# The turns of w_out and the gates' folds inside the first block's steps, and an opening with long products: linear attention and two expert layers on one core

## The reference

```python
for t in range(S):                       # B=4, H=8, S=768, D=48
    cur = np.einsum('bhd,bhe->bhde', u[None] * kt, vt)
    y[:, :, t] = np.einsum('bhd,bhde->bhe', rt, state + cur)
    state = w[None, :, :, None] * state + np.einsum('bhd,bhe->bhde', kt, vt)
x = y as 3072 tokens x 384
h = max(x @ w1, x @ w2, x @ w3)          # 384 -> 768
x = h @ w_out                            # 768 -> 384
logits = x @ w_gate;  noisy = logits + log1p(exp(x @ w_noise)) * noise
top 2 of 8 experts, softmax over the two; out += weight * relu(x @ ew1[e]) @ ew2[e]
```

## Time and profile before

| | us |
|---|---|
| median of 3 runs | 889.2 |
| the profiled execution, its own time | 889.12 |
| its span | 887.2 |
| TensorE busy | 872.6 (98%) |
| VectorE busy | 451.0 (51%) |
| ScalarE busy | 271.2 (31%) |
| POOL busy | 385.2 (43%) |
| mean granted clock of TensorE | 0.994 |

### The profile page before, as it was taken

How to read it: one execution, slowest core, us unless ns; L and a number is a source line. 1 busy time by engine, 2 the same in 40 slices (tenths; PEclk the granted TensorE clock), 3 DMA queues, 4 the chain that set the end, 5 groups by cost and what they waited for, 6 DMA issues and landing times. The chain is left out here.

```text
span 887.2 us, 19589 instructions
## 1 busy us (share of the span) xinstructions
PE 872.6 (98%) x6566; PEld 855.1 (96%) x6567; DVE 451.0 (51%) x1100; ACT 271.2 (31%) x520; POOL 385.2 (43%) x380
## 2 busy tenths in 40 slices
PE   7999999999999999999999999999999999999996
PEld 6999999999999999999999999999999999999996
DVE  6675555636564564646573564352525335264322
ACT  3442322223231233215314342331414233143210
POOL 5245244244253534325444555454534435355442
PEclk9899999999999999999999999999999999999999
DMA  9595212222122221023215622624326252442221
GB/s 229 132 293 138 68 51 64 60 58 58 57 57 61 57 64 37 2 92 97 46 46 190 176 77 50 187 61 142 116 60 199 70 180 73 137 135 69 64 78 52
DMA packets 103765, 86.08 MB, mean 97 GB/s; under 512 B 60634, under 2 KB 93090, under 8 KB 103696
## 3 DMA queue, kind: packets, MB, share of 16 engines
q1 hardware_dynamic: 82704, 31.56, 15.0%
q0 software_dynamic: 12416, 26.28, 9.6%
q10 hardware_dynamic: 8576, 27.33, 9.5%
HBM read 70.46 MB, written 21.35 MB: 103 GB/s over the span
## 5 line engine op out<-in xcount | busy, mean ns | idle before, releaser
L1413 PE MATMUL ps<-yh,wh 128*128 128x384 f32 x432 | 148.7, 344 | 1.7 <-ACT x_sb L1196 1.3
L1304 ACT ACTIVATE gh<-ps 128x384 fp32r<-128x384 f32 x136 | 66.9, 492 | 264.6 <-PE ps L1415 264.6
L1415 PE MATMUL ps<-yh,wl 128*128 128x384 f32 x432 | 145.5, 337 | 0.0
L1414 PE MATMUL ps<-yl,wh 128*128 128x384 f32 x432 | 145.4, 337 | 0.0
L1413 PE MATMUL ps<-xgh,w1h 128*128 128x384 f32 (+1 forms) x456 | 145.0, 318 | 0.0
L1415 PE MATMUL ps<-xgh,w1l 128*128 128x384 f32 (+1 forms) x456 | 145.0, 318 | 0.0
L1414 PE MATMUL ps<-xgl,w1h 128*128 128x384 f32 (+1 forms) x456 | 144.9, 318 | 0.0
L1060 DVE SCALAR_TENSOR_TENSOR gl<-ps,gh 128x384 fp32r<-128x384 f32 x136 | 75.8, 557 | 126.8 <-ACT gh L1304 126.8
L1413 PE MATMUL ps<-w2h,gh 128*128 128x384 f32 x408 | 138.2, 339 | 0.6 <-DVE gl L1054 0.6
L1414 PE MATMUL ps<-w2l,gh 128*128 128x384 f32 x408 | 136.5, 335 | 0.0
L1415 PE MATMUL ps<-w2h,gl 128*128 128x384 f32 x408 | 136.5, 335 | 0.0
(11 more groups left out here) (200 smaller groups left out, 1497.1 us busy)
## 6 DMA issues: line engine op xcount, KB each, us to landing
ew_raw<-ew ACTq DMA_DIRECT2D x28, 768.0 KB, 4.6
v_sb<-vN SPq DMA_DIRECT2D x24, 192.0 KB, 3.3
out<-zrow SPq DMA_DIRECT2D x1, 4608.0 KB, 16.3
x_rows<-x_sb ACTq DMA_DIRECT2D x8, 576.0 KB, 3.6
kn_sb<-kN SPq DMA_DIRECT2D x20, 192.0 KB, 2.8
k_raw<-kT SPq DMA_DIRECT2D x48, 72.0 KB, 2.7
wraw<-moe_w SPq DMA_DIRECT2D x6, 576.0 KB, 6.9
e_raw<-ew SPq DMA_DIRECT2D x4, 768.0 KB, 5.0
```

The source lines that it names most:

```text
L1304: act.activation(gh[:, f, :], ps[f % 4][:, 0:T], ACT.Relu).then_inc(gh_ok, 1)
L1413: pe.matmul(o, ah, bh, start=start, stop=False)
L1414: pe.matmul(o, ah, bl, start=False, stop=False)
L1415: return pe.matmul(o, al, bh, start=False, stop=stop)
```

## The change

1. The opening's 22 transposes of the identity become 4 products of 384 columns: the identity by `state[0]`, which POOL has cleared, so the result is zero. Three transposes follow, and further groups of 4, 3, 8, 6 and 6 are put between the chunks' parts. `keep_turning` now takes a bank.
2. `turn_wo(0)` moves from behind the second own sums to the end of the opening, `turn_wo(1)` behind the first block's step 0. Both use banks 7, 6 and 3. ScalarE keeps the second half in step 0, behind the first maxima, and TensorE waits for all six parts (`wo_ok`) behind step 1.
3. Both folds move behind the block's step 3 (bank 6, beyond column 384), ScalarE's copy and split of them with them, VectorE's `fold_low` from behind step 3 to behind step 4.
4. SyncE's queue loads the first three weight pieces ahead of w_out. The first piece is split earlier: by ScalarE ahead of its parts of y, by VectorE between the second and third chunk's rows.
5. The third chunk's own sums stand ahead of the second outputs, on TensorE and VectorE.
6. Buffers are laid out in another order in SBUF; no size changes.

```diff
 TURN = (6, 7, 0)
-FOLD = 1
+WO_TURN = (7, 6, 3)
+FOLD = 6
...
+            for q in range(BS):
+                load_piece(q)
             for n in range(2):
                 at = 3 * KD * F1 + n * PW
                 sp.dma_start(wo_raw[n][:, :, :].rearrange("p f n -> p (f n)"), moe_w[:, at:at + PW]).then_inc(wo_in[n], 16)
-            for q in range(BS):
-                load_piece(q)
...
                 if first:
-                    fold_low(0)
-                    fold_low(1)
                     split_wo_low(0)
...
                 if first:
+                    fold_low(0)
+                    fold_low(1)
                     split_wo_low(1)
...
             masks(0, 2)
+            own_weights(0, 2)
             states(0, 1)
             rows_of_y(0, 1)
-            own_weights(0, 2)
             split_y_low(0, 0, 3)
+            split_piece_low(0)
             rows_of_y(0, 2)
             split_y_low(0, 1, 4)
             split_y_low(0, 2, 0)
-            split_piece_low(0)
             states(0, 2)
...
-                    if first and f == 2:
+                    if first and f == 0:
+                        keep_turned(1)
+                    if first and f == 3:
+                        keep_folded()
                         split_fold_high(0)
                         split_fold_high(1)
...
             fade(0, 1)
-            keep_turned(0)
-            keep_turned(1)
+            split_piece_high(0)
             split_y_high(0, 0, 3)
             split_y_high(0, 1, 4)
             split_y_high(0, 2, 0)
-            split_piece_high(0)
-            keep_folded()
+            keep_turned(0)
             fade(0, 2)
...
                 if n == 0:
-                    pe.wait_ge(nat_ok, 1)
-                    pe.wait_ge(mask_ok, 4)
+                    pe.wait_ge(a_ok, 3)
+                    pe.wait_ge(yn_ok, 3)
+                    pe.wait_ge(yl_ok, 1)
...
                     hidden(i, f)
+                    if first and f == 0:
+                        turn_wo(1)
+                    if first and f == 1:
+                        pe.wait_ge(wo_ok, 2 * KD)
+                    if first and f == 3:
+                        pe.wait_ge(gate_in, 16)
+                        pe.wait_ge(yn_ok, BS + 1)
+                        fold(0)
+                        fold(1)
+                    if first and f == 4:
+                        pe.wait_ge(fold_ok, 1)
...
             pe.wait_ge(const_ok, 1)
-            keep_turning(22)
+
+            for _ in range(4):
+                pe.matmul(ps[7][:, 0:DM], ident[:, :], state[0][:, :, :].rearrange("p q n -> p (q n)"), start=True, stop=True)
+            keep_turning(3, 7)
...
             products(0, 0)
+            keep_turning(4, 7)
             own_sums(0, 0)
+            keep_turning(3, 6)
             products(0, 1, 1)
             outputs(0, 0)
             products(0, 2)
             own_sums(0, 1)
-            turn_wo(0)
-            turn_wo(1)
+            pe.wait_ge(nat_ok, 1)
+            keep_turning(8, 0)
+            own_sums(0, 2)
             outputs(0, 1)
-            own_sums(0, 2)
             pe.wait_ge(mask_ok, 6)
             turn_y(0, 0, 3)
+            keep_turning(6, 0)
             outputs(0, 2)
             turn_y(0, 1, 4)
-            pe.wait_ge(gate_in, 16)
-            fold(0, range(1))
+            keep_turning(6, 0)
             turn_y(0, 2, 0)
-            fold(0, range(1, 3))
-            fold(1, range(3))
-            pe.wait_ge(fold_ok, 1)
+            turn_wo(0)
             period(0, 0, 1, True, False, first=True)
```

More of the change, by code:

```diff
@@ L167, in build @@
         hmax = [sb(f"hmax{i}", [P, BT], where=turn2) for i in range(3)]
+        hh = sb("hh", [P, F1T, BT], F32R, where=turn2)
+        hl = sb("hl", [P, F1T, BT], F32R, where=turn2)
         turn3 = ExitStack()
@@ L170, in build @@
         turn3.close()
-        hh = sb("hh", [P, F1T, BT], F32R, where=turn2)
-        hl = sb("hl", [P, F1T, BT], F32R, where=turn2)
         turn3 = ExitStack()
         x_sb = sb("x_sb", [P, BS, WO], where=turn3)
-        route = sb("route", [P, 8, BS, NE], where=turn3)
+        spread = sb("spread", [P, 5, NE, NTILE], where=turn3)
+        plan_f = sb("plan_f", [P, 4, NE + 1], where=turn3)
         best = sb("best", [P, BS, NE], where=turn3)
         best_i = sb("best_i", [P, BS, NE], U32, where=turn3)
+        route = sb("route", [P, 8, BS, NE], where=turn3)
         onehot = sb("onehot", [P, BS, 2, NE], where=turn3)
@@ L185, in build @@
         zrow = sb("zrow", [P, DM], where=turn3)
-        plan_f = sb("plan_f", [P, 4, NE + 1], where=turn3)
-        spread = sb("spread", [P, 5, NE, NTILE], where=turn3)
         tile_f = sb("tile_f", [P, 2, NTILE], where=turn3)
@@ L211, in folded @@
         def folded(n):
-            return ps[FOLD][:, n * 6 * NE:(n + 1) * 6 * NE].rearrange("p (f e) -> p f e", f=3)
+            return ps[FOLD][:, DM + n * 6 * NE:DM + (n + 1) * 6 * NE].rearrange("p (f e) -> p f e", f=3)
         w_in, gate_in, noise_in = sem("w_in"), sem("gate_in"), sem("noise_in")
@@ L1152, in keep_turned @@
                     act.wait_ge(wo_mm, KD * n + k + 1)
-                    act.activation(woT[n][:, k, :], ps[k][:, 0:BT], ACT.Copy).then_inc(wo_ok, 1)
+                    act.activation(woT[n][:, k, :], ps[WO_TURN[k]][:, 0:BT], ACT.Copy).then_inc(wo_ok, 1)
             def keep_folded():
                 act.wait_ge(fold_mm, 1)
-                act.activation(fold_sb[:, :, :], ps[FOLD][:, 0:12 * NE].rearrange("p (f e) -> p f e", f=F1T), ACT.Copy).then_inc(fold_ok, 1)
+                act.activation(fold_sb[:, :, :], ps[FOLD][:, DM:DM + 12 * NE].rearrange("p (f e) -> p f e", f=F1T), ACT.Copy).then_inc(fold_ok, 1)
             def split_fold_high(n):
@@ L1474, in turn_wo, with fold @@
                     for f in range(3):
-                        mm = pe.transpose(ps[k][:, f * P:(f + 1) * P], wo_raw[n][:, f, k * P:(k + 1) * P], ident[:, :])
+                        mm = pe.transpose(ps[WO_TURN[k]][:, f * P:(f + 1) * P], wo_raw[n][:, f, k * P:(k + 1) * P], ident[:, :])
                     mm.then_inc(wo_mm, 1)
-            def fold(n, slices):
-                pe.wait_ge(wo_ok, 2 * KD)
-                for f in slices:
+            def fold(n):
+                for f in range(3):
                     for k in range(KD):
@@ L1519, in period, with keep_turning @@
                 x_product(i, 2)
-            def keep_turning(n):
+            def keep_turning(n, bank):
                 for _ in range(n):
-                    pe.transpose(ps[7][:, 0:P], ident[:, :], ident[:, :])
+                    pe.transpose(ps[bank][:, 0:P], ident[:, :], ident[:, :])
             pe.wait_ge(const_ok, 1)
-            keep_turning(22)
+            for _ in range(4):
+                pe.matmul(ps[7][:, 0:DM], ident[:, :], state[0][:, :, :].rearrange("p q n -> p (q n)"), start=True, stop=True)
+            keep_turning(3, 7)
             pe.wait_ge(wkn_ok, 1)
```

## The result

Measured side by side, 19 runs each: **890.98 us** (888.53 to 892.23) against 887.6 us (883.81 to 889.7) before, ratio **1.0034** [1.0023, 1.0046]. The change makes the kernel a little slower. The forecast of 886.9 us was 4 us too low and had the wrong sign; the range just holds the median. The profiled execution took 890.73 us, 1.61 us more than the one of before.

The account below looks back on a forecast made before the run. The prediction took TensorE to be bound by a stream of products after 47.6 us, so its start and the work put into it decide. From 889.1 us, -6.3 for the earlier start and +4.1 for folds gave 886.9 us, range 884.8 to 891.0.

Parts of the forecast that it names:

- I lean to no fall: At the folds inside the block: the clock stays up behind the 36 passes, so no cost; chance 0.48 for the forecast.
- Part 1: Kernel start: long products take 5.1 us plus 0.7 for three transposes, hidden in TensorE's idle time; cost 0 to 1 us.
- may give: Kernel start: the long products have the full clock up when the work behind `wkn` begins, around 10 us.
- Part 2: Opening at the full clock: VectorE sets the pace, second outputs at 20.8 us, block begins at about 28.9 us.
- the 6.7 us: Opening: the block begins that much earlier, at about 28.9 us instead of 35.62.
- Part 3: Block's first product to fourth chunk's products: late partners, a new `woT` wait of some 1.7 us, products at 41.3 us.
- the -6.3 us: Gain at the start of the fourth chunk's products: 41.3 us instead of 47.62.
- Part 4: Folds inside the block's stream: 36 passes that nothing hides, +4.1 us, bounds 3.6 to 4.7.
- rival A: Behind the folds: the clock falls again, costing 3.1 us on full products, for 890.0 us; chance 0.30.
- D: Opening of the kernel before: its clock rose early in some runs, so the difference may shrink to nothing; no share.
- B: Opening, 10 to 24 us: the clock is not up or does not stay, 4.5 us, for 891.4 us; chance 0.12.
- C: Wait on `woT` before the fourth chunk's products: 1.7 us shorter, folds 0.5 us cheaper, for 884.7 us; chance 0.10.

Follow-up runs that it names:

- after_again: The changed kernel itself, measured again on the third chip: 896.66 us, ratio 1.0025 to the kernel before.
- a_22: Changed kernel with the old 22 transposes in place of its 4 long products and 3 transposes: 895.9 us, ratio 1.0037 to the kernel before.
- b_short: Kernel before plus 6 and 5 short transposes in TensorE's two opening waits, its 22 transposes kept: 891.19 us, ratio 0.9968.
- b_hold: Kernel before with 4 long products and 3 transposes for the 22, plus 6 and 5 short transposes in two opening waits: 891.0 us, ratio 0.9974.
- b_hold_again: The same kernel as b_hold, measured on the third chip beside the changed kernel: 890.18 us, ratio 0.9955 to the kernel before.
- a_thirdfold: Changed kernel leaving out 12 of its 18 folds, so gate columns differ from the reference: 875.29 us, ratio 0.986 to the kernel before.
- a_split: Changed kernel with nine folds behind the block's step 2 and nine behind step 3, same work: 888.53 us, ratio 1.0016 to the kernel before.
- a_noshort: Changed kernel without the 27 short transposes between the chunks' parts: 890.48 us, ratio 1.0036 to the kernel before.
- a_fold0: Changed kernel with nine folds behind the block's step 0 and nine behind step 3: 893.01 us, ratio 1.000 to the kernel before.
- c_fill: Changed kernel with w_out's turns and loads back in the opening, nine folds before the block, nine behind step 0: 888.04 us, ratio 0.9942 to before.
- c_again: The same kernel as c_fill, measured on the third chip beside the changed kernel: 888.26 us, ratio 0.9933 to the kernel before.
- b_long: Kernel before with 4 long products and 3 transposes in place of the 22 transposes, nothing else: 885.94 us, ratio 0.9989.

## Why the prediction was wrong, step by step

The step that failed is the one that the prediction calls deciding: "I lean to no fall". It put the fall of the clock behind the folds at nothing, and it cost 3.2 us. A second mistake goes with it: the gain was counted against one execution with a rare late rise, while most runs of before, by their mean clocks, have no such moment.

**Part 1, the long products.** The price was right: 8 passes took 5.49 us in after_again, where the level rose only at their end, for 5.1 forecast, and in the changed kernel's first profile they ended ahead of `wkn` as said. What they "may give" was not theirs. It was read from one execution, in which 22 transposes raised nothing; in a_22 and b_short the level was up at 8.54 and 7.49 us behind the same transposes. What an engine's clock does in one execution was taken for what the kernel does.

**Part 2, the opening at full clock.** Right in its marks: block start 29.08 for 28.9 us, second outputs 21.07 for 20.8 us, VectorE setting the pace. But the 6.7 us were counted from an execution whose level rose only in the turns of `wo_raw`. Against kernels with the early rise (b_hold 31.11, b_short 31.26) the opening is 2.0 to 2.2 us shorter; b_hold_again's 32.45 us has 3 us at the low level in its folds.

**Part 3, to the fourth chunk's products.** The wait on `woT` came, 1.04 us instead of 1.7. Two things were missed ahead of it: `wl` at 3.62 us instead of 2.6, priced from a row without POOL beside it, and the wait for the maxima that follows from it, 0.99 us. So it is 42.09 us instead of 41.3, and against the profiled execution of before **the -6.3 us measured -5.5**. Against a kernel with the early rise they are nearly nothing: b_hold, with turns and folds left in the opening, has these products at 42.26 us. The block starts 2 us earlier and only 0.2 us of it is left at 42 us: 13.0 us for the two steps against 11.15, although 3.4 us of b_hold's lie at the low level. Nearly all of the 5.5 us are the late rise of one execution, and not the work of the moves.

**Part 4, the folds.** 4.32 us in the row (4.1 in after_again) for 4.1 forecast, and paid in full (a_thirdfold). The way from the fourth chunk's products to the x products says 3.9: 32.05 us in a_split against 28.18 in b_hold and in before, which have no folds there. That most of the first row was at full clock, as the prediction took it, holds.

**What decides.** "I lean to no fall" was wrong. All four profiled executions with the 36 passes inside the block (the changed kernel twice, a_22, a_noshort) fell at or behind them, and of the changed kernel's 19 runs two have a mean clock of 0.999 while the rest have 0.992 to 0.997. The fall costs 3.2 us, as priced under rival A (3.1). The argument against it was that full products on both sides and a shorter stretch would protect the clock. They did not protect it behind a group of 36. Behind groups of 18 no profile shows a fall (a_split, a_fold0, c_fill, c_again). a_split has all 36 passes with a step of products between its halves, so what counts is that they stand together, as far as the mean clocks of its unprofiled runs bear it out.

**The sum against the measured time.** From 886.9: +3.2 the fall, +0.8 the partners' chain, -0.2 the folds (3.9 us for 4.1) is 890.7 us; the profiled execution took 890.73.

**The sign.** The fall and the choice of what to measure against each take the gain away. Without the fall, a_split's profiled execution took 887.76 us: less than the 889.12 us of before that the sums started from, as forecast, but its median is still 1.0016 [1.0001, 1.003] of before. The median of before is 887.6 us over 19 runs, 1.5 us under that execution. With the fall the changed kernel is slower than both.

**The sum against before.** After b_hold's marks: 2.0 us gained at block start, 1.9 lost again by 42 us, then 35.26 us to the x products against 28.18, which is 3.9 for the folds and 3.2 for the fall: 7 us in all, 77.35 against 70.44. b_hold pays for a fall as well, but its stretch is 3.41 us long and lies at the block's start (an estimate by rival A's rates: 3.41 x (1 - 0.173/0.320) = 1.6 us, inside its 11.15). In the profiled execution of before, 1.55 of the 6.8 us lie ahead of the block, on the end of the folds and a wait. So moving the folds inside did not remove the fall, and put all 6.8 us of it inside the block.

**The rivals.** A held, with its 890.0 us, at 0.30 against the forecast's 0.48. D held in substance too and was given no share, because it moves the time of before and not of the changed kernel. B did not come in the changed kernel (no run of 19 has a mean clock under 0.992), and a_noshort shows that it could have: 13.65 us at the low level. The Trainium skill, page "TensorE: Matmul & The Clock Gate", Part 4 (PE-mode transpose), by which the full clock does not engage for transpose mode, is contradicted by b_short and a_22: 22 transposes in a row were enough. C did not come: its wait was shorter, but the chain ahead of it longer. The range was added up a little wrong: by its own terms it goes from 884.7 (886.9 - 1.7 - 0.5) to 891.6 us (890.0 + 0.6 + 1), and the median lies in either.

**What stays open.** Why the level rises behind the same 22 transposes at 8 us in most executions and behind 21.7 us in a few, and which of the opening's waits lets it fall in a given run; the traces show the levels, not the reason. Whether the long products prevent the rare late rise is not shown either: a_22 and b_short show no clear sign of one in 24 runs without them. That the 13 runs of before at 0.988 to 0.990 fell in the opening is read from their mean clock and from the traces of b_long and a_noshort; no execution of before that fell there was profiled. The order of the loads and the earlier split of the first weight piece were not tested by themselves. And why TensorE waits behind the first block on the second and third chip and not on the first is not known.

## What to carry to other kernels

Before costing a change that is to mend something seen in one profiled execution, look at the spread of the runs and their mean clocks: the worst moment of a trace may be a rare one, and the gain then as well. The same holds the other way: an execution without a fall, as that of a_fold0, may be the rare one. Work moved out of an opening with waits into a stream without them is paid in full, and can bring a fall of the clock along; here it did better in waits that remained, in two pieces, as in c_fill. A partner's instruction that is moved beside another engine's work may take longer, here by a third to six tenths.

## What the hardware showed that I had not expected

- The clock fell while TensorE was busy all the time: in the four profiles with 36 passes of 16 columns inside the block (4.1 to 4.4 us) the level went to 1.2 GHz at or behind them, for 3.4 to 6.8 us. Behind 18 passes in 2.08 us it did not, in eight stretches of four profiles (a_split, a_fold0, c_fill, c_again).
- In b_long and a_noshort it fell in waits of about 1 us between short groups of products, and a few transposes of a constant in these waits, 11 in b_short, were worth 0.3%.
- VectorE's subtraction of 128x1152 took 1.3 us alone and 1.8 with POOL at work beside it (2.1 in a_split, 4.26 us for two). POOL was slower as well: `k_upd` took 0.99 us alone and 1.79 beside it, and 2.12 in c_fill.
